# Lead-in by head, and rounding of query, key and value moved to GpSimd, in an attention and MLP kernel

## Reference

```python
q_rot, k_rot = (rotate(q), rotate(k))          # x1*cos - x2*sin, x1*sin + x2*cos
scores = scale * np.matmul(q_rot, k_rot.transpose(0, 1, 3, 2))
attn = np.exp(scores - np.max(scores, axis=-1, keepdims=True))
attn = attn / (np.sum(attn, axis=-1, keepdims=True) + 1e-09)
x = np.matmul(attn, v)                         # heads side by side: (4, 576, 512)
h = x.transpose(0, 2, 1) @ U @ V
u = x + h.transpose(0, 2, 1)
out = u + np.maximum(u @ w_ch1, 0.0) @ w_ch2
```

## Time and profile before

| what | us |
|---|---|
| median of three runs | 781.98 |
| the profiled execution | 785.53 |
| its span | 783.7 |
| PE busy | 719.9 (92%) |
| ACT busy | 448.2 (57%) |
| POOL busy | 455.3 (58%) |
| DVE busy | 405.0 (52%) |

### The profile page before, as it was taken

The page is one execution under the profiler, slowest core; times in us unless marked ns, Lnnn a source line. Parts: engine busy times, 40 slices in busy tenths (PEclk is TensorE's granted clock), DMA queues, the critical chain, the costliest instruction groups (busy, mean ns, idle before and its releaser), DMA issues.

```text
span 783.7 us, 12244 instructions
## 1 busy us (share of the span) xinstructions
PE 719.9 (92%) x4252; PEld 645.1 (82%) x4252; DVE 405.0 (52%) x669; ACT 448.2 (57%) x959; POOL 455.3 (58%) x349
## 2 busy tenths in 40 slices
PE   0888888799999999999999999999999699999998
PEld 0777776689999787989899988889999579899896
DVE  2687887665555776444454456565554642112111
ACT  1787886567576766555565565666665333333332
POOL 2565667348576775485584876647533226556553
PEclk9999998699999999999999999999999999999999
DMA  7966566453656635727547265282622135345342
GB/s 236 238 163 164 144 165 196 105 164 100 203 143 211 148 118 160 230 81 208 177 136 238 91 187 169 95 235 72 175 90 96 41 128 167 134 156 171 126 162 80
DMA packets 74700, 119.59 MB, mean 153 GB/s; under 512 B 27152, under 2 KB 27280, under 8 KB 72848
## 3 DMA queue, kind: packets, MB, share of 16 engines
q1 hardware_dynamic: 73600, 116.98, 50.1%
q10 hardware_dynamic: 1040, 1.84, 0.8%
HBM read 81.04 MB, written 9.44 MB: 115 GB/s over the span
## 4 chain that ended last, share of the span: by engine, by line
PE 75%; DVE 9%; ACT 6%; issue 4%; DMA 3%; POOL 2%; ACTq 0%; POOLq 0%; DVEq 0%; SPq 0%
PE ps L927 23%; PE ps L945 22%; PE ps L855 9%; PE ps L842 8%; PE ps L875 7%; DVE negmax L705 2%; ACT prob L569 2%; PE ps L868 1%; DVE ptl L713 1%; DVE pth L717 1%; PE ps L909 1%; ACT pth L579 1%; DMA sin_t<-in_sin 1%; DMA stack<-raw 1%; PE ps L897 1%
## 5 line engine op out<-in xcount | busy, mean ns | idle before, releaser
L495 POOL TENSOR_TENSOR w1l<-w1u,w1h 128x512 fp32r<-128x512 f32 x96 | 124.0, 1292 | 245.1 <-ACT w1h L610 245.1
L705 DVE TENSOR_REDUCE negmax<-ps 128x1 f32<-128x576 f32 (+1 forms) x160 | 120.3, 752 | 82.5 <-PE ps L842 80.2
L579 ACT ACTIVATE pth<-ps 128x512 fp32r<-128x512 f32 (+1 forms) x192 | 107.7, 566 | 90.0 <-PE ps L875 88.0
L788 DVE SCALAR_TENSOR_TENSOR htl<-ps,hth 128x384 fp32r<-128x384 f32 x96 | 53.5, 557 | 186.1 <-ACT hth L621 185.9
L842 PE MATMUL ps<-stack 128*128 128x288 f32 (+1 forms) x640 | 119.6, 310 | 22.9 <-DMA stack<-raw 21.5
L569 ACT ACTIVATE prob<-ps,negmax 128x576 f32<-128x576 f32 (+1 forms) x160 | 118.0, 738 | 38.6 <-DVE negmax L705 38.2
L927 PE MATMUL ps<-uth,w1h 128*128 128x384 f32 x384 | 132.8, 346 | 0.7 <-DVE utl L779 0.5
L927 PE MATMUL ps<-uth,w1l 128*128 128x384 f32 x384 | 129.9, 338 | 0.0
L927 PE MATMUL ps<-utl,w1h 128*128 128x384 f32 x384 | 129.7, 338 | 0.0
L621 ACT ACTIVATE hth<-ps 128x384 fp32r<-128x384 f32 x96 | 47.2, 491 | 139.9 <-PE ps L927 139.7
L501 POOL TENSOR_TENSOR w2l<-w2u,w2h 128x512 fp32r<-128x512 f32 x96 | 123.7, 1289 | 4.5 <-ACT w2h L614 4.5
(11 more groups left out here) (60 smaller groups left out, 1074.8 us busy)
## 6 DMA issues: line engine op xcount, KB each, us to landing
w1u<-in_w SPq DMA_DIRECT2D x96, 256.0 KB, 2.7
w2u<-in_w SPq DMA_DIRECT2D x96, 256.0 KB, 2.7
stack<-raw SPq DMA_DIRECT2D x64, 288.0 KB, 4.2
raw<-in_qk SPq DMA_DIRECT2D x14, 1152.0 KB, 5.4
stack<-raw SPq DMA_DIRECT2D x60, 144.0 KB, 3.9
v2u<-in_v SPq DMA_DIRECT2D x16, 320.0 KB, 3.8
res<-scratch_u SPq DMA_DIRECT2D x18, 256.0 KB, 3.5
out<-res SPq DMA_DIRECT2D x18, 256.0 KB, 2.2
```

Of the source, the lines that this page charges most:

```text
L495: nc.gpsimd.tensor_tensor(w1l[:, at], w1u[:, at], w1h[:, at], ALU.subtract).then_inc(w1_lo, 1)
L579: nc.scalar.activation(pth[rows, keys, queries], source, ACT.Copy).then_inc(pt_hi, 1)
L705: nc.vector.tensor_reduce(negmax[0:WT[t], t:t + 1], scores_of(n, WT[t]), AX.XY, ALU.max, negate=True).then_inc(maxed, 1)
L788: nc.vector.scalar_tensor_tensor(htl[:, i % 2], up_bank(), 0.0, hth[:, i % 2], ALU.max, ALU.subtract).then_inc(relu_lo, 1)
```

## The change

1. Lead-in by head. The loads of q and k and of the tables are cut by partitions: first the 64 rows of head 0 (k, then q), then the 64 rows of head 1 in one transfer each. Cosine and sine lie in one array, so that one product of 1152 elements in a row takes the place of two of 576. DVE ropes and splits head 0's k and q and then head 1's; the product of head 1's k stands ahead of the rest of head 0's q. Each head is stacked when its own parts are ready.
2. Order of loads. q of pair 1 is loaded at once behind head 1; k of pair 1 and v of pair 0 behind the stack transfers of k. Loads of later pairs are two transfers, q and k. U and V are loaded, rounded and split ten slots later.
3. POOL no longer waits for DVE's rests in the lead-in; it waits for the tables and its own rows. Its rope is two operations (one product of 1152, one sum).
4. For pairs 1 to 5 POOL also rounds q, k and v, with the rests directly behind; ACT does this for pairs 6 to 15 as before.
5. v of pair 0 is rounded by ACT in slot 2 and its rest is taken by DVE in slot 3, not by POOL.

```diff
-FIRST_V = 1
+FIRST_V = 2
+POOL_ROUNDS = range(1, 6)
...
-            sp.dma_start(raw[:, 0, :, 1], qk[0][:, :, 1]).then_inc(first_loaded, 16)
-            sp.dma_start(raw[:, 0, :, 0], qk[0][:, :, 0]).then_inc(raw_loaded[0], 16)
-            sp.wait_ge(raw_loaded[0], 16)
-            sp.dma_start(raw[:, 1, :, 0], qk[1][:, :, 0]).then_inc(raw_loaded[1], 16)
-            sp.wait_ge(lo_split[1], 1)
+            for which in (1, 0):
+                sp.dma_start(raw[0:D, 0, :, which], qk[0][0:D, :, which]).then_inc(lead_loaded[which], 16)
+            sp.dma_start(raw[D:P, 0], qk[0][D:P]).then_inc(lead1_loaded, 16)
+            load(1, 0)
+            sp.wait_ge(lead_lo[0][1], 1)
             stack_k(sp, 0, 0)
-            sp.wait_ge(lo_split[0], 1)
-            sp.dma_start(raw[:, 1, :, 1], qk[1][:, :, 1]).then_inc(first_loaded, 16)
+            sp.wait_ge(lead_lo[1][1], 1)
+            stack_k(sp, 0, 1)
+            load(1, 1)
             load_v(0)
-            stack_k(sp, 0, 1)
-            load_v(1)
...
             def rope(r, which):
-                x, xs = raw[:, r % 2, 0, which], raw[:, r % 2, 1, which]
-                nc.gpsimd.tensor_tensor(x, x, cos_t[:, which], ALU.mult).then_inc(chain, 1)
-                done[0] += 1
-                link(nc.gpsimd.tensor_tensor(xs, xs, sin_t[:, which], ALU.mult))
-                nc.gpsimd.tensor_tensor(x, x, xs, ALU.add).then_inc(roped[which], 1)
+                both = raw[:, r % 2, :, which]
+                link(nc.gpsimd.tensor_tensor(both, both, tables[:, :, which], ALU.mult))
+                nc.gpsimd.tensor_tensor(both[:, 0], both[:, 0], both[:, 1], ALU.add).then_inc(roped[which], 1)
+                if r in POOL_ROUNDS:
+                    pool.wait_ge(roped[which], r)
+                    nc.gpsimd.tensor_copy(both[:, 1].bitcast(F32R), both[:, 0]).then_inc(qk_hi[which], 1)
+                    split_lo(r, which)
...
+                if r in POOL_ROUNDS:
+                    if r == 1:
+                        pool.wait_ge(v_split, 1)
+                    pool.wait_ge(v_loaded[r % 2], 16 * (r // 2 + 1))
+                    nc.gpsimd.tensor_copy(v2[:, r % 2, :, :, 0], v2u[:, r % 2, :, :, 1]).then_inc(v_hi, 1)
...
-            pool.wait_ge(k_tables, 32)
-            pool.wait_ge(q_tables, 32)
-            for which in range(2):
-                pool.wait_ge(lo_split[which], 1)
+            pool.wait_ge(lead_tables[1], 16)
+            pool.wait_ge(lead_tables[0], 16)
+            pool.wait_ge(tables_loaded, 16)
             prepare(1, ROPE_Q)
             prepare(1, ROPE_K)
-            split_v(0)
...
-            split_qk(0, 1)
-            split_qk(0, 0)
-            act.wait_ge(lo_split[0], 1)
-            for j in range(2):
-                stack_q(act, 0, j)
+            for which in (1, 0):
+                act.dma_start(tables[0:D, :, which], cos_sin[0:D, :, which]).then_inc(lead_tables[which], 16)
+            act.dma_start(tables[D:P], cos_sin[D:P]).then_inc(tables_loaded, 16)
             act.dma_start(ident[:, :], identity).then_inc(ident_loaded, 16)
+            for which in (1, 0):
+                first_hi(slice(0, D), which, lead_roped[0][which], lead_hi[0][which])
+            act.wait_ge(lead_lo[0][0], 1)
+            stack_q(act, 0, 0)
+            for which in (1, 0):
+                first_hi(slice(D, P), which, lead_roped[1][which], lead_hi[1][which])
+            act.wait_ge(lead_lo[1][0], 1)
+            stack_q(act, 0, 1)
...
-                if n == NT:
+                if n == 3 * NT:
                     act.wait_ge(mix_loaded, 32)
...
+            first_products(head0, 1)
+            first_sum(head0, 1, 1, lead_roped[0][1])
...
+            first_products(head0, 0)
+            first_lo(head0, 1, lead_hi[0][1], lead_lo[0][1])
+            first_sum(head0, 0, 2, lead_roped[0][0])
+            dve.wait_ge(tables_loaded, 16)
+            dve.wait_ge(lead1_loaded, 16)
+            first_products(head1, 1)
+            first_lo(head0, 0, lead_hi[0][0], lead_lo[0][0])
+            first_sum(head1, 1, 3, lead_roped[1][1])
+            first_products(head1, 0)
+            first_lo(head1, 1, lead_hi[1][1], lead_lo[1][1])
+            first_sum(head1, 0, 4, lead_roped[1][0])
+            first_lo(head1, 0, lead_hi[1][0], lead_lo[1][0])
...
+                if n == FIRST_V + 1:
+                    dve.wait_ge(v_hi, 1)
+                    nc.vector.tensor_tensor(v2[:, 0, :, :, 1], v2u[:, 0, :, :, 1], v2[:, 0, :, :, 0],
+                                            ALU.subtract).then_inc(v_split, 1)
```

More of the change, by code:

```diff
@@ L205, in build @@
         ident = sb("ident", [P, P])
-        cos_t, sin_t = sb("cos_t", [P, 2, S]), sb("sin_t", [P, 2, S])
+        tables = sb("tables", [P, 2, 2, S])
+        cos_t, sin_t = tables[:, 0], tables[:, 1]
         raw = sb("raw", [P, 2, 2, 2, S])
@@ L262, in _engines @@
 def _engines(nc, e):
-    (qk, v, cos, sin, identity, u4, v4, w, scratch_u, out, bank_of, before, left) = (e[x] for x in (
-        "qk v cos sin identity u4 v4 w scratch_u out bank_of before left").split())
-    (ps, ident, cos_t, sin_t, raw, stack, v2u, v2, prob, pth, ptl, low, xt, negmax, sums, inv, xn, xh, xl, hsum, hs, us, vs,
+    (qk, v, cos_sin, identity, u4, v4, w, scratch_u, out, bank_of, before, left) = (e[x] for x in (
+        "qk v cos_sin identity u4 v4 w scratch_u out bank_of before left").split())
+    (ps, ident, tables, cos_t, sin_t, raw, stack, v2u, v2, prob, pth, ptl, low, xt, negmax, sums, inv, xn, xh, xl, hsum, hs, us, vs,
      uth, utl, w1h, w1u, w1l, w2h, w2u, w2l, hth, htl, res, uraw, vmraw) = (e[x] for x in (
-         "ps ident cos_t sin_t raw stack v2u v2 prob pth ptl low xt negmax sums inv xn xh xl hsum hs us vs "
+         "ps ident tables cos_t sin_t raw stack v2u v2 prob pth ptl low xt negmax sums inv xn xh xl hsum hs us vs "
          "uth utl w1h w1u w1l w2h w2u w2l hth htl res uraw vmraw").split())
-    (k_tables, q_tables, ident_loaded, first_loaded, mix_loaded, mix_consts, zeroed, raw_loaded, v_loaded, first_rope,
+    (lead_tables, lead_loaded, lead_roped, lead_hi, lead_lo, tables_loaded, ident_loaded, lead1_loaded, mix_loaded, mix_consts, zeroed, raw_loaded, v_loaded, first_rope,
      chain, roped, qk_hi, lo_split, v_hi, v_split, stacked, scored, maxed, expd, transposed, pt_hi, pt_lo, pv_done,
@@ L339, in stacked_pair, with load @@
                     sp.wait_ge(stacked[g % HEADS_STACKED], STACKED * (g // HEADS_STACKED + 1))
-            def load(r):
-                if r >= 2:
+            def load(r, which):
+                if r >= 2 and which == 0:
                     stacked_pair(r - 2)
-                sp.dma_start(raw[:, r % 2], qk[r]).then_inc(raw_loaded[r % 2], 16)
+                sp.dma_start(raw[:, r % 2, :, which], qk[r][:, :, which]).then_inc(raw_loaded[r % 2][which], 16)
             def load_v(r):
@@ L359, in stack_pair @@
                     if j == 0:
[L360 removed]
+                        sp.wait_ge(lo_split[1], r)
                     stack_k(sp, r, j)
@@ L422, in _ @@
                     stack_pair(r + 1)
[L423 to L426, removed]
+                if n == STACK:
+                    load(2, 1)
                     sp.dma_start(uraw, u4).then_inc(mix_loaded, 16)
                     sp.dma_start(vmraw, v4).then_inc(mix_loaded, 16)
+                if s == LOAD and r + 3 < NPAIRS:
+                    load(r + 3, 0)
+                    load(r + 3, 1)
+                if n == 0:
+                    load(2, 0)
+                    load_v(1)
                 for b, what, t in mixes_of(n - STORE_LAG):
@@ L482, in prepare @@
                     split_v(r)
-                if s == SPLIT_K + 1:
+                if s == SPLIT_K + 1 and r not in POOL_ROUNDS:
                     split_lo(r, 1)
@@ L646, in _ @@
                         lower_half(*half)
-                if r + 1 < NPAIRS:
+                if r + 1 < NPAIRS and r + 1 not in POOL_ROUNDS:
                     if s == SPLIT_Q:
@@ L673, in _ @@
         def _(dve):
[L674 to L696, removed]
@@ L697, in _, with first_products, first_sum @@
-            first_sum(0)
-            first_lo(0)
+            def first_products(rows, which):
+                both = raw[rows, 0, :, which]
+                nc.vector.tensor_tensor(both, both, tables[rows, :, which], ALU.mult).then_inc(first_rope, 1)
+            def first_sum(rows, which, nth, made):
+                dve.wait_ge(first_rope, nth)
+                nc.vector.tensor_tensor(raw[rows, 0, 0, which], raw[rows, 0, 0, which], raw[rows, 0, 1, which],
+                                        ALU.add).then_inc(made, 1)
@@ new lines, in first_lo @@
+            def first_lo(rows, which, rounded, made):
+                dve.wait_ge(rounded, 1)
+                nc.vector.tensor_tensor(raw[rows, 0, 0, which], raw[rows, 0, 0, which], raw[rows, 0, 1, which],
+                                        ALU.subtract).then_inc(made, 1)
+            head0, head1 = slice(0, D), slice(D, P)
```

(4 more changed lines are left out.)

46 lines of the change are left out of this document (25 added, 21 removed).

## The result

The changed kernel took 790.92 us (median of four runs, 790.62 to 794.71); the kernel before, with one more run beside these, 783.79. The ratio is 1.010, 95% interval 1.0066 to 1.0134. The forecast was 783.9, with a range to 788: too low, and outside the range. The profiled execution took 790.9, its span is 789.1, 5.4 us over the 783.7 of before.

The account below looks back on a forecast made before the run. PE was taken to set the end from 160 us on, so early gains or losses pass through whole. Terms +3.8 - 0.4 + 1.2 - 2.7 = +1.9 us on the median 781.98 gave 783.9, range 777 to 788.

Parts of the forecast that it names:

- U's and V's rounding moves ten slots ... 0: Rounding of U and V: its 1.4 us on ACT cost some 0.4 in either place, so 0.
- the rule: DVE operations with two SBUF operands and POOL operations reading SBUF hold each other up; up to 0.98 us for one operation.
- Pair 0 ... -0.4: Slots 1 and 2: 2.90 us falls to 1.8 without roundings, v's rounding returns 0.73 in slot 2; -0.4 us.
- The lead-in, +3.8: Up to the first exponential: slow loads and POOL taking turns with DVE move it from 23.67 to 27.5; +3.8 us.
- the picture of the halves: Lead-in loads: 64 partitions at 198 GB/s, two queues for a while filling lower and upper rows together; all in at 14.3.
- my main case: Lead-in with slow loads, POOL getting in at DVE's first pause, 18.5; sum +1.9 us, 783.9, chance 0.45.
- the case without it: Lead-in with slow loads and neither POOL nor DVE holding the other: first exponential at 23.3, -0.4 us.
- v's rest, +1.2: Pair 0, v's rest on DVE while POOL ropes k of pair 1, held for half its product; +1.2 us, 0 to 3.5.
- POOL's rounding, -2.7: Pairs 1 to 5: ACT loses roundings, 0.57 in slots 13, 23, 33, 43, 0.13 in slot 3, 0.3 in 46; -2.7 us.
- The lock in full: Rival: POOL and DVE take turns from 16.4 in the lead-in (+5.7), v's rest fully held (+3.5); 788.5, chance 0.12.
- The rival of fast halves: Lead-in: 64-partition loads run at 381 GB/s, POOL still in DVE's way; -3.2 us, 778.8, chance 0.20.
- the one of nothing in the way: Rival: POOL and DVE run side by side without holds; 774.4 with fast loads, 778.5 with slow; chance 0.15.

Follow-up runs that it names:

- e6: The changed kernel with the rests of U and V on POOL instead of DVE, in the same slot; 788.47 us (one run).
- e10: The changed kernel with lead-in loads over 128 partitions, POOL waiting for DVE's last lead-in rest, and U's and V's rests on POOL; 779.75 us, ratio to before 0.994.
- e4: The changed kernel with ACT loading head 1's tables before head 0's, so both partition halves fill at once; 793.62 us (one run).
- e1: The changed kernel, but POOL again waits for DVE's last rest of the lead-in before roping pair 1; 786.13 us, ratio to before 1.002.
- e5: The kernel before with only POOL's rounding of q, k and v of pairs 1 to 5 added; 783.97 us, ratio to before 0.9992.

## Why the prediction failed, by its own steps

The forecast was 7.0 us too low. If the medians beside the experiments are taken as the kernel before, half of it (3.5) lies in the number that the sum was put on, and half in the sum: 5.5 measured, 1.9 forecast.

- **"U's and V's rounding moves ten slots ... 0".** This is the step that failed. It priced ACT's two roundings, rightly (slot 5 is 0.38 shorter, slot 15 is 0.34 longer), and never asked what runs on POOL when DVE's two rests come in slot 16. V's rest took 3.10 us for 0.75: +2.36, and 0.13 in slot 17 (e6: slot 16 falls to 2.29). I had applied the rule in the lead-in and to v's rest, and not to this third place of the same kind.
- **"Pair 0 ... -0.4".** From 2.90 us with two roundings and 1.8 without I took 1.1 off slot 1. It stayed at 3.06 with no rounding on ACT; tiles 0 to 2 take 3.79 in both kernels. What ends it is PE, as these two rows of the changed kernel have it (the scores that slot 2's row maximum waits for, and those of tile 15):

```profile
29.59 1.31 PE L874 MATMUL ps<-stack 128*128 128x288 f32 x4
...
57.57 0.79 PE L874 MATMUL ps<-stack 128*128 128x288 f32 x4
```

  The same four matmuls take 1.31 us near the start and 0.79 later, before and after. The clock column reads 1.00 there. But in e10 the same four take 1.31 us too, in a stretch that the column has at the lower level:

```profile
35.00:36.00 1.00, 1.00 (x7) 1.00 (x6) 0.00 (x0) 0.46 (x2) 1.00 (x2) 0.50 1.01 205
35.56 1.31 PE L873 MATMUL ps<-stack 128*128 128x288 f32 x4
```

  So the matmuls near the start, behind a lead-in that has hardly any, take as long as at 1.2 GHz, and the forecast compared slot 1 with slots at the upper level. The transposes ahead of them are long as well (1.11 for 0.66). The two together are an estimated 0.97 of the 1.1 us. With v's rounding back in slot 2 (+0.48) the term is +0.48 where -0.4 was forecast.
- **The lead-in, +3.8.** Measured 4.27: the mechanism was right, the nearness in part luck. Head 1's tables landed at 14.4 (taken: 14.3, from the picture of the halves that e4 refutes), POOL started at 16.4 (15.9), first exponential 27.94 (27.5). They took turns from 16.4 on, with all four of POOL's operations in DVE's chain. That was not my main case (POOL in at 18.5) but the one that I had priced at 29.4, +5.7. It came out 1.5 us cheaper, since the copy is short (0.66 us alone in slot 17 of the changed kernel; taken: 1.0) and a held operation ends about 0.6 us behind the other, not its full 0.75. e1 gives 4.7 for the lost wait alone; the sum for the case without it had -0.4, and e1 has -0.41 (23.26), within the 1.1 us by which the old lead-in itself varies.
- **v's rest, +1.2.** Slot 3 is +1.08, but by another operation than I had: v's rest (34.15, 2.04 us) stood behind POOL's sum (34.09 to 35.50), not in the middle of its product. The size was luck.
- **POOL's rounding, -2.7.** Mis-sized: about -1.6. -0.57 in each of slots 13, 23, 33, 43, as worked out (e5, too). But slot 46's -0.33 is given back by slot 47's +0.33, slots 15, 25 and 35 are some 0.1 longer each and slots 44 and 45 0.40 together, in e5 as in the changed kernel. A pair takes 19.44 us (slots 20 to 29) where 19.3 was forecast. What ends the waits in those slots I did not follow.
- **The clock.** The profiled execution before had a half-clock stretch in slot 26 that the changed one had not: 1.58 in favour of the change. The miss of the profiles, 5.37 against 1.9, is 3.5: 2.5 (slots 16, 17) + 0.9 (pair 0) + 1.1 (POOL's rounding) + 0.5 (lead-in) - 0.1 (v's rest), less 1.6 for the clock, and 0.2 that I did not follow.
- **The zero.** I put the sum on a median of three runs, 781.98. The 25, 17 and 15 runs of it beside the experiments have medians of 785.35, 785.45 and 785.44. Against that the change costs 5.5 us, as by the profiles (against the four runs beside its own it is 7.1); a forecast from the profiled execution's own 785.53 would have been 787.4, still 3.5 too low.

The lock in full, my rival on the slower side at 788.5, had the right mechanism and the right order in the lead-in, a price there that was too high (5.7 for 4.27), and the wrong second place: v's rest instead of V's. The rival of fast halves fell with the loads (some 210 to 240 GB/s), the one of nothing in the way with DVE's 3.06 us.

## What to carry to other kernels

When work moves to GpSimd, or a wait between GpSimd and VectorE goes, list every VectorE operation with two operands in SBUF in the whole stage and ask what GpSimd runs beside each; a longer (merged) GpSimd operation makes each hold longer (3.10 us beside one of 1152, 1.88 beside one of 576). A wait that seems to protect nothing may be keeping two engines apart. Price an operation by the engine that ends the wait in its own slot, not by a slot elsewhere with TensorE at another pace. And a zero from three runs is not good enough for a forecast of 0.5%.

## What the runs showed of the hardware

- A VectorE operation with two SBUF operands that meets a running GpSimd operation lasts until that ends and then some 0.6 us, where it takes 0.75 alone: 3.06 with a product of 2.61, 1.84 with one of 1.56. GpSimd is held the same way: its cast of 576 took 1.68 in the lead-in and 0.66 when alone. A VectorE operation with one operand in PSUM was not held: L741 took 0.68 at 33.43, beside a product from 31.37 to 34.01.
- Loads from HBM to 64 partitions moved at 208 to 240 GB/s (stretches of 3 us in the changed kernel) where 128 partitions moved at 380 to 401, and two at once, one to each half, at 212 together.
- GpSimd casts 128x576 float32 to float32r in 0.66 us, less than half of its 1.41 for two operands; ScalarE needs 0.68.
- Four matmuls of 128x288 take 0.79 us at a granted clock of 1.00 and 1.31 at 0.50. They take 1.31 as well right behind the lead-in, where the clock column reads 1.00: there it can't be relied on.
